# Seven block products for eight with w2 and wo, in parts of 512 tokens

## The reference

```python
h = (x.T @ U @ V).T              # rank 32, over the sequence
u = x + h
out = u + relu(u @ w1) @ w2      # x: [1536, 512], w1: [512, 2048], w2: [2048, 512]
```

## Time and profile before

| | us |
|---|---|
| median of three runs | 456.3 |
| the profiled execution, its own time | 455.48 |
| its span, first to last instruction | 453.7 |
| last stage, 236.30 to 450.20 | 213.9 |

### The profile page before, as it was taken

How to read it: one execution, slowest core, us unless ns; L and a number is a source line. 1 busy time by engine, 2 the same in 40 slices (tenths; PEclk the granted TensorE clock), 3 DMA queues, 4 the chain that set the end, 5 groups by cost and what they waited for, 6 DMA issues and landing times.

```text
span 453.7 us, 8487 instructions
## 1 busy us (share of the span) xinstructions
PE 441.6 (97%) x3194; PEld 367.8 (81%) x3194; DVE 188.5 (42%) x615; ACT 166.4 (37%) x451; POOL 174.8 (39%) x247
## 2 busy tenths in 40 slices
PE   4999999999999999999999999999999999999996
PEld 3677777887787887667998888888888888888885
DVE  5799998265533634553351222221222122222112
ACT  4898886142643644756331011111012101111102
POOL 0777788806951555775011212222211121122210
PEclk9999999999999999999999999999999999999999
DMA  8797981100020011110101011110111022311003
GB/s 264 231 278 241 265 247 48 49 2 0 4 93 0 1 48 48 46 48 1 48 23 48 25 46 46 48 44 29 46 46 48 2 92 92 94 47 48 25 0 139
DMA packets 29949, 33.47 MB, mean 74 GB/s; under 512 B 9204, under 2 KB 19444, under 8 KB 29908
## 3 DMA queue, kind: packets, MB, share of 16 engines
q1 hardware_dynamic: 29474, 32.40, 23.9%
q10 hardware_dynamic: 434, 0.52, 0.3%
HBM read 29.77 MB, written 3.15 MB: 73 GB/s over the span
## 4 chain that ended last, share of the span: by engine, by line
PE 95%; ACT 1%; DMA 1%; issue 1%; DVE 1%; SPq 0%; POOL 0%; ACTq 0%
PE ps_s L1209 27%; PE ps_o L1209 25%; PE ps_t L1209 12%; PE ps_t L1241 5%; PE ps_s L1228 5%; PE ps_o L1261 5%; PE ps_s L1440 5%; PE ps_o L1473 4%; PE ps_t L1456 4%; PE ps_o L1385 1%; DMA kT<-in_k 1%; DVE prob L844 0%; ACT probT L681 0%; PE ps_o L1374 0%; ACT prob L609 0%
## 5 line engine op out<-in xcount | busy, mean ns | idle before, releaser
L495 POOL TENSOR_TENSOR fl<-fraw,fh 128x512 fp32r<-128x512 f32 x32 | 41.3, 1292 | 177.9 <-DVE fh L1151 177.9
L793 ACT ACTIVATE hidh<-ps_o 128x768 fp32r<-128x768 f32 x32 | 26.0, 813 | 175.8 <-PE ps_o L1209 175.8
L609 ACT ACTIVATE prob<-prob,smin 128x256 f32<-128x256 f32 (+3 forms) x144 | 77.6, 541 | 33.5 <-DVE smin L844 32.8
L1192 DVE SCALAR_TENSOR_TENSOR hidl<-ps_o,hidh 128x768 fp32r<-128x768 f32 x32 | 30.6, 957 | 93.0 <-ACT hidh L793 93.0
L545 POOL TENSOR_SCALAR prob<-prob,sinv,one 128x256 f32<-128x256 f32 (+1 forms) x96 | 50.5, 540 | 24.3 <-DVE sinv L875 24.1
L572 POOL TENSOR_SCALAR prob<-prob,sinv,gate 128x128 f32<-128x128 f32 (+5 forms) x48 | 34.0, 717 | 53.0 <-DVE sinv L895 52.9
L1209 PE MATMUL ps_s<-hidh,fl 128*128 128x512 f32 x128 | 50.4, 394 | 0.0
L1209 PE MATMUL ps_s<-hidl,fh 128*128 128x512 f32 x128 | 50.2, 392 | 0.0
L1209 PE MATMUL ps_s<-hidh,fh 128*128 128x512 f32 x128 | 49.7, 388 | 0.0
L1151 DVE CAST fh<-fraw 128x512 fp32r<-128x512 f32 x32 | 14.4, 449 | 66.5 <-PE ps_t L1209 66.4
L1209 PE MATMUL ps_o<-xh,w_late 128*128 128x512 f32 (+1 forms) x160 | 41.6, 334 | 0.0
(11 more groups left out here) (180 smaller groups left out, 976.8 us busy)
## 6 DMA issues: line engine op xcount, KB each, us to landing
fraw<-in_w SPq DMA_DIRECT2D x32, 256.0 KB, 2.6
wraw<-in_w SPq DMA_DIRECT2D x8, 512.0 KB, 3.3
kT<-in_k SPq DMA_DIRECT2D x16, 224.0 KB, 3.8
vN<-in_v SPq DMA_DIRECT2D x8, 384.0 KB, 4.1
out<-prob SPq DMA_DIRECT2D x12, 256.0 KB, 2.7
qT<-in_q SPq DMA_DIRECT2D x7, 384.0 KB, 3.3
vB<-in_v SPq DMA_DIRECT2D x8, 192.0 KB, 4.2
kT<-in_k SPq DMA_DIRECT2D x7, 128.0 KB, 3.4
```

What stands on the lines that cost most here:

```text
L495: return pool.tensor_tensor(lo, raw, hi.bitcast(F32), ALU.subtract)
L609: act.activation(prob_s, prob_s, ACT.Exp, bias=smin[:, col:col + 1], scale=-1.0, accum_out=ssum[:, col:col + 1]).then_inc(done, 1)
L793: act.activation(hidh[:, f % 2, :], ps_o[:, 0:S], ACT.Relu).then_inc(hidh_done, 1)
L1192: dve.scalar_tensor_tensor(hidl[:, f % 2, :], ps_o[:, 0:S], 0.0, hidh[:, f % 2, :].bitcast(F32), ALU.max, ALU.subtract).then_inc(hidl_done, 1)
```

## The change

The output product of the last stage is cut in 2 x 2 blocks and done with seven block products (Strassen's scheme in Winograd's form) where eight stood. A block of weights is 128 x 256 (half of a pair of 128-row tiles, by half of the 512 output features), a block of data 128 rows by 256 tokens. The 1536 tokens fall into 3 parts of 512; a pair `g` is two tiles of 128 rows of `w2` (8 pairs) or `wo` (pair 0 of a part), so 27 pairs.

For each made pair: one DMA of 512 KB into `fraw`; VectorE makes four sums of blocks (`weights_combined`); ScalarE rounds three blocks and the four sums (`weights_hi`, `combined_weights_hi`); VectorE makes both low halves. Five places hold the split weights: pairs 0 and 1 stay in two of them for all parts, the other seven pairs of a part take turns in three and are made again in each part. For each pair's data: Relu to `hraw` in fp32, four sums (`combined_first`, `combined_others`), rounding on ScalarE (`hidden_hi`, `combined_hi`), low halves on VectorE (`hidden_lo`, `combined_lo`). GpSimd does none of it. The seven products accumulate in seven PSUM banks over a part; then six sums and one subtraction on VectorE and one copy on ScalarE make the four output blocks. Buffers of the stage lie over ones of earlier stages; the splits of `wo` on GpSimd (and `WO_BEHIND`) go.

```diff
+TOKENS, BLOCK = 512, 256
...
+PAIRS = FT // 2 + 1
+N_PAIR = PARTS * PAIRS
...
+PRODUCTS = {1: ("a11", "b11"), 2: ("a12", "b21"), 3: ("s4", "b22"), 4: ("a22", "t4"), 5: ("s1", "t1"), 6: ("s2", "t2"),
+            7: ("s3", "t3")}
+ORDER, END_ORDER = (1, 2, 3, 5, 7, 6, 4), (1, 6, 7, 5, 2, 3, 4)
+SUM_AT = {"u2": 1, "u3": 2, "c22": 3, "u4": 4, "c11": 5, "c12": 6, "c21": 7}
...
+KEPT, TURNS = 2, 3
...
+        banks = {1: ps_s[:, 0, :], 2: ps_s[:, 1, :], 3: ps_s[:, 2, :], 4: ps_s[:, 3, :], 5: ps_o[:, 512:1024],
+                 6: ps_t[:, 0, :], 7: ps_t[:, 1, :]}
...
+            for g in range(N_PAIR):
...
                     sp.wait_ge(mpv_done, M_UNIT)
...
+                if m >= 2:
+                    sp.wait_ge(al_done, 2 * (m - 1))
+                if c and j == 4:
+                    store(c - 1)
+                src = t["w2"][2 * j - 2:2 * j].rearrange("f p n -> p f n") if j else t["wo"]
+                sp.dma_start(fraw[:, m % 2, :, :].rearrange("p (f h) n -> p f (h n)", f=2), src).then_inc(f_in[m % 2], 16)
+            store(PARTS - 1)
...
-                lo_of(fraw[:, f % 2, :], fh[:, f % FR, :], fl[:, f % FR, :]).then_inc(fl_done, 1)
...
+            def weights_hi(g):
...
+                    act.wait_ge(*end_of(c * PAIRS + j + KEPT))
+                act.activation(a_hi3[a_place(g)], fraw[:, m % 2, 1:4, :], ACT.Copy).then_inc(ah_done, 1)
+            def combined_weights_hi(g):
+                act.wait_ge(s_step, 4 * (made_before(g) + 1))
+                act.activation(a_hi4[a_place(g)], sraw[:, :, :], ACT.Copy).then_inc(ah_done, 1)
+            def hidden_out(g, f):
+                n = 2 * hidden_before(g) + f
+                act.wait_ge(hid_done, n + 1)
+                if hidden_before(g):
+                    act.wait_ge(b1l_done, hidden_before(g))
+                act.activation(hraw[:, 2 * f:2 * f + 2, :], ps_o[:, 0:TOKENS].rearrange("p (s n) -> p s n", s=2),
+                               ACT.Relu).then_inc(relu_done, 1)
+            def hidden_hi(g):
+                act.wait_ge(relu_done, 2 * hidden_before(g) + 2)
...
+                act.activation(b1_hi[g % 2], hraw[:, 1:4, :], ACT.Copy).then_inc(b1h_done, 1)
+            def combined_hi(g):
+                act.wait_ge(t_step, 4 * (g + 1))
...
+                act.activation(bt_hi[g % 2], t_raw, ACT.Copy).then_inc(bth_done, 1)
+            def copy_first(c):
...
+                act.wait_ge(acc_done, 7 * c + END_ORDER.index(1) + 1)
+                act.activation(p1, banks[1], ACT.Copy).then_inc(copy_done, 1)
...
+            weights_hi(0)
+            combined_weights_hi(0)
...
+                if last_of_part(g):
+                    copy_first(g // PAIRS)
+                    if g + 1 < N_PAIR:
+                        combined_hi(g + 1)
...
+                    hidden_out(g + 1, 0)
+                    if makes:
+                        weights_hi(g + 2)
+                    hidden_out(g + 1, 1)
+                    hidden_hi(g + 1)
+                    if makes:
+                        combined_weights_hi(g + 2)
+                    combined_hi(g + 1)
...
+            def weights_combined(g):
...
+                a21, a11, a22, a12 = (fraw[:, m % 2, n, :] for n in range(4))
+                s1, s2, s3, s4 = (sraw[:, n, :] for n in range(4))
+                dve.wait_ge(f_in[m % 2], 16 * (m // 2 + 1))
...
+                dve.tensor_tensor(s1, a21, a22, ALU.add).then_inc(s_step, 1)
+                dve.tensor_tensor(s3, a11, a21, ALU.subtract).then_inc(s_step, 1)
+                dve.wait_ge(s_step, 4 * m + 1)
+                dve.tensor_tensor(s2, s1, a11, ALU.subtract).then_inc(s_step, 1)
+                dve.wait_ge(s_step, 4 * m + 3)
+                dve.tensor_tensor(s4, a12, s2, ALU.subtract).then_inc(s_step, 1)
+            def weights_lo(g):
...
+                dve.wait_ge(ah_done, 2 * m + 1)
+                dve.tensor_tensor(a_lo3[a_place(g)], fraw[:, m % 2, 1:4, :], a_hi3[a_place(g)].bitcast(F32),
+                                  ALU.subtract).then_inc(al_done, 1)
+            def combined_weights_lo(g):
+                dve.wait_ge(ah_done, 2 * made_before(g) + 2)
+                dve.tensor_tensor(a_lo4[a_place(g)], sraw[:, :, :], a_hi4[a_place(g)].bitcast(F32),
+                                  ALU.subtract).then_inc(al_done, 1)
...
+            def combined_first(g):
+                b12, b11, _, _ = hidden_blocks(g)
...
+                    dve.wait_ge(relu_done, 2 * hidden_before(g) + 1)
...
+                    dve.wait_ge(sum_done, OP_PIECES[1] if g else OP_PIECES[0])
+                if g:
+                    dve.wait_ge(btl_done, g)
+                dve.tensor_tensor(t_raw[:, 0, :], b12, b11, ALU.subtract).then_inc(t_step, 1)
+            def combined_others(g):
+                b12, b11, b22, b21 = hidden_blocks(g)
+                t1, t2, t3_, t4 = (t_raw[:, n, :] for n in range(4))
...
+                    dve.wait_ge(relu_done, 2 * hidden_before(g) + 2)
+                dve.tensor_tensor(t3_, b22, b12, ALU.subtract).then_inc(t_step, 1)
+                dve.wait_ge(t_step, 4 * g + 1)
+                dve.tensor_tensor(t2, b22, t1, ALU.subtract).then_inc(t_step, 1)
+                dve.wait_ge(t_step, 4 * g + 3)
+                dve.tensor_tensor(t4, t2, b21, ALU.subtract).then_inc(t_step, 1)
+            def hidden_lo(g):
+                dve.wait_ge(b1h_done, hidden_before(g) + 1)
+                dve.tensor_tensor(b1_lo[g % 2], hraw[:, 1:4, :], b1_hi[g % 2].bitcast(F32),
+                                  ALU.subtract).then_inc(b1l_done, 1)
+            def combined_lo(g):
+                dve.wait_ge(bth_done, g + 1)
+                dve.tensor_tensor(bt_lo[g % 2], t_raw, bt_hi[g % 2].bitcast(F32), ALU.subtract).then_inc(btl_done, 1)
+            def whole(c, n):
+                dve.wait_ge(acc_done, 7 * c + END_ORDER.index(n) + 1)
+            def first_sum(c):
...
+                dve.wait_ge(copy_done, c + 1)
+                whole(c, 6)
+                dve.tensor_tensor(u2, banks[6], p1, ALU.add).then_inc(sum_step, 1)
+            def other_sums(c):
...
+                whole(c, 7)
...
+                dve.tensor_tensor(u3, banks[7], u2, ALU.add).then_inc(sum_step, 1)
+                whole(c, 5)
...
+                dve.tensor_tensor(y22, banks[5], u3, ALU.add).then_inc(sum_step, 1)
+                dve.tensor_tensor(u2, banks[5], u2, ALU.add).then_inc(sum_step, 1)
+                whole(c, 2)
+                dve.tensor_tensor(y11, banks[2], p1, ALU.add).then_inc(sum_step, 1)
+                whole(c, 3)
...
+                dve.tensor_tensor(y12, banks[3], u2, ALU.add).then_inc(sum_step, 1)
+                whole(c, 4)
+                dve.scalar_tensor_tensor(y21, banks[4], -1.0, u3, ALU.mult, ALU.add).then_inc(sum_step, 1)
...
+            weights_combined(0)
             for n in range(OP_PIECES[0]):
                 mixed_lo(n)
             w01_lo(4)
             t3_lo(1)
+            weights_lo(0)
+            combined_weights_lo(0)
+            combined_first(0)
+            combined_others(0)
             w01_lo(5)
             mixed(0)
             mixed(1)
-            f_hi(0)
+            combined_lo(0)
+            weights_combined(1)
             w01_lo(6)
             mixed_lo(OP_PIECES[0])
             mixed_lo(OP_PIECES[0] + 1)
-            f_hi(1)
+            weights_lo(1)
+            combined_weights_lo(1)
             w01_lo(7)
...
+            for g in range(N_PAIR):
+                makes = g + 2 < N_PAIR and is_made(g + 2)
+                if not last_of_part(g):
+                    if makes:
+                        weights_combined(g + 2)
+                    combined_first(g + 1)
+                    if makes:
+                        weights_lo(g + 2)
+                    combined_others(g + 1)
+                    hidden_lo(g + 1)
+                    if makes:
+                        combined_weights_lo(g + 2)
+                    combined_lo(g + 1)
...
+                    if g + 1 < N_PAIR:
+                        combined_first(g + 1)
+                        combined_others(g + 1)
+                    first_sum(g // PAIRS)
+                    if g + 1 < N_PAIR:
+                        combined_lo(g + 1)
+                    other_sums(g // PAIRS)
...
+            def hidden(g, f):
...
+                n = 2 * hidden_before(g) + f
+                if c == 0:
+                    pe.wait_ge(w01l_done, j)
+                if j == 1:
+                    pe.wait_ge(opl_done, OP_PIECES[1] if c else OP_PIECES[0])
+                if n:
+                    pe.wait_ge(relu_done, n)
                 else:
                     pe.wait_ge(sum_done, OP_PIECES[1])
...
-            def second(f):
-                pe.wait_ge(hidl_done, f + 1)
-                pe.wait_ge(fl_done, f + 1)
...
-                for m, k in order:
-                    w, cols = slice(m * P, (m + 1) * P), PIECES[k]
-                    last = split_product(u_piece(m, k),
```

(50 more changed lines are left out.)

307 lines of the change are left out of this document (166 added, 141 removed).

## The result

| | before | after |
|---|---|---|
| median of 4 runs, us | 456.27 (456.04 to 457.19) | 440.65 (439.81 to 441.42) |
| profiled execution, us (span) | 455.48 (453.7) | 440.83 (439.0) |

Timed again later beside other kernels, the changed kernel took 441.92 us, ratio 0.9692 [0.967, 0.9715], so two timings of one kernel differ by 0.3%. Differences between experiments are read with that in mind.

What follows compares the result with a forecast made beforehand. TensorE, busy all 213.90 us of the last stage, was taken as the bound: 453.7 - 18.5 + 1.2 + 2.8 + 0.6 = 439.8 us span, 441.6 with 1.8 around it, median 442.4 us; range 438 to 452.

Steps and rivals of the forecast that it cites:

- Columns, −18.5: Last stage, TensorE: 331,776 columns removed, 290,304 added; balance -41,472 at 0.4456 ns each, -18.5 us.
- Layout, +1.2: Stage's 1,134 product matmuls, 256 wide: spacing depends on where tiles lie, 0.113 to 0.1187 us against 0.114; +1.2 us taken.
- The forecast's lower bound: Fast end of the layout term: 1,134 product matmuls at 0.113 instead of 0.114 us, given as -1.3 us.
- Waits, +2.8: TensorE stalls: stage start +1.2 and 0.1 for restarting, three part ends 0.5 each, +1.5 us.
- VectorE 6.98 of 7.53 us: Steady step making a pair's weights: VectorE needs 6.98 us of TensorE's 7.53, margin 0.55 us, no steady-state stall.
- Rival 1: VectorE's back-to-back overlap is lost: 7.94 us per step, VectorE the bound, 453 us; chance, whole or part, 0.15.
- rival 3: VectorE and ScalarE take turns: steps above 8.2 us make the kernel slower, 510 us if no copies covered; chance 0.07.
- Signs of being right: Steady steps 7.5 us apart, TensorE idle only near 246 and at part ends, VectorE about 90% busy for 55 us.
- Kept weights: Two weight sets kept on chip save VectorE work in parts 2 and 3 that was within its margin: nothing.
- GpSimd leaves, 0: Last stage: GpSimd's 40.1 us there were hidden beside TensorE, so its leaving gains nothing.
- Tail, +0.6: Kernel end: six VectorE sums in a row end 1.2 us after TensorE instead of 0.64, +0.6 us.
- Profile to median, +0.8: Whole kernel: profiled execution lay 0.8 us below the three-run median of 456.3, so 441.6 became a 442.4 us median.

Runs made afterwards that it cites:

- late low halves: Changed kernel with the two low halves of the second batch's mixed output moved from before the first step to the seventh: 439.49 us, 0.9645; control 0.9692.

## Why the prediction was right, and where it was off

By its own steps, in the profiled execution's span (453.7 to 439.0 is −14.7, forecast −13.9):

- **Columns, −18.5.** Right in mechanism and price: the steady step is 7.50 us (7.53 forecast) and TensorE has no gap in it. The stage lost 16.0 us: 18.5 of columns, with 2.8 of waits added and 0.3 of layout taken off.
- **Layout, +1.2.** Too much, and for a reason that the traces don't bear out. From 236.96 to where a next matmul would have started (434.60 + 0.11 = 434.72) are 197.8 us. At the 0.4460 ns per column of the whole stage before (213.76 us for its 479,232 columns) 437,760 columns are 195.3, and the waits by starts are 2.8 (next item). That leaves −0.3 us. (The forecast's lower bound, 1,134 x (0.113 − 0.114), is −1.1 and not −1.3.) The prediction put the slow spacing of the earlier trace rows down to where the tiles lie. That alone doesn't decide it. In both kernels the slow stretch of the earlier trace rows goes on over the first matmuls on `xh` and `woT` and turns fast on the same tiles, at 234.14 us before and 234.80 after. And the same matmuls on the same tiles ran 0.35 us per three (0.118 each) in the changed kernel after its wait at 299 us, the first fence, and 0.34 (0.113 each) in the kernel with the late low halves, the second:

```profile
299.60 0.50 PE L1469 MATMUL ps_t<-b_parts,a_third 128*128 128x256 f32 x2 [0.21 <-DVE b_parts L1373]
299.94 0.28 PE L1469 MATMUL ps_t<-b_parts,a_third_low 128*128 128x256 f32 x1
...
300.29 0.28 PE L1469 MATMUL ps_t<-b_parts,a_third_low 128*128 128x256 f32 x1
```

```profile
298.04 0.28 PE L1470 MATMUL ps_t<-b_parts,a_third_low 128*128 128x256 f32 x1
...
298.38 0.28 PE L1470 MATMUL ps_t<-b_parts,a_third_low 128*128 128x256 f32 x1
```

- **Waits, +2.8.** 2.8: the start 1.31 + 0.08 = 1.39 (1.3 forecast), the part ends 3 x 0.48 = 1.45 (1.5). Right in place, cause and size; by the prediction's own numbers `hidden_lo(1)` ends at 246.5, not 246.4, which makes the start 1.3 + 0.1. The experiment with the late low halves shows the cause of the first.
- **VectorE 6.98 of 7.53 us.** Measured alone: 6.94, with three terms of every product cut to two. The price line through the 512- and 768-column rows held for 256 (0.42) and 1,024 (1.22). Rival 1 would have been 7.94, rival 3 over 8.2; both are ruled out by the 6.94 us steps.
- **Signs of being right.** VectorE is busy for 14.86 of the 15 us from 247 to 262 and 21.58 of the 24 from 270 to 294, after it has caught up. About 90% was said for the first 55 us of the stage; from 236.3 to 294 us it was 95%, so this sign was set too low, against the prediction's own 6.98 of 7.53 us (93%) and the backlog in front.
- **Kept weights "nothing either": wrong.** 7 to 8 us. The step failed because it used the margin of a step in the steady state. The work of pairs 9, 10, 18 and 19 would fall into a part's last two steps and the next one, where TensorE has 4.8 us for one step and VectorE 3.9 us of sums besides. The change keeps these weights, so the forecast time didn't suffer from it.
- **GpSimd leaves, 0.** Right for what was removed. It would have been wrong to reason from it that GpSimd is a free place to put work: with the low halves of the weights there it cost about 33 us. Before, VectorE was idle for 164 of 214 us here, so GpSimd had room beside it; now it has not.
- **Tail, +0.6.** 0.8: the last sum ends 1.4 us after TensorE, not 1.2; the time from there to the end is 0.1 shorter.
- **Head.** Not in the sum: TensorE reached the stage at 236.96 instead of 236.30, +0.7. It varies from run to run, from 236.0 to 238.6 us in the traces of the experiments, whose code ahead of the stage is almost the same. The wait for `kT`'s load is 0.7 us longer than before here (3.6 and 2.9), but in other traces the two don't go together (3.9 us with the stage at 236.44, 3.8 with 238.58), so the cause stays open.
- **Profile to median, +0.8: wrong.** The profiled execution of before lay 0.8 under its median, that of after 0.2 over it. This is 1.0 of the 1.7 us of the miss; a difference of one profiled run from its median is chance and should not be carried over. The rest, 0.8 us of span, is the layout (1.5 too much), of which the head, by luck, gave 0.7 back.

## What to carry to other kernels

Before a trade of TensorE columns for VectorE work, add up VectorE's step from its start-to-start spacings, not durations, and compare it with TensorE's new step; do it once more for each irregular step (the first, the last of a part, the one after), for there a margin of 7% is nothing. A margin that is sized for an average step says nothing of a step with a third less TensorE work. To judge an edit of 1 us, compare the stage alone in the traces as well as the medians. Don't move two-input work to GpSimd to relieve a VectorE that is nearly full: it takes VectorE's time as well as its own.
